# An attention and MoE kernel: heads laid out in four classes, the 64-row attention products in turns over four 64x64 quarters in place of two

## What is computed

```python
# attention, per head: state is 48 x 48
k_n = k / (norm(k) + 1e-6)
for t in range(768):
    y[t] = q[t] @ state
    v_old = k_n[t] @ state
    state = state + beta[t] * outer(k_n[t], v[t] - v_old)
# first MoE, all 3072 tokens, 384 -> 768 -> 384
x = maximum(maximum(y @ w1, y @ w2), y @ w3) @ w_out
# second MoE: noisy gate, top 2 of 8 experts, 384 -> 1024 -> 384
```

## Time and profile before

| | |
|---|---|
| median of 3 runs | 1016.75 us (1013.34 to 1016.77) |
| profiled execution, span from first to last instruction | 1010.6 us |
| TensorE busy | 990.2 us, 98% of the span |
| VectorE, ScalarE, GpSimd busy | 727.5, 464.6, 218.4 us |
| share of the chain that ended last | TensorE 92%, VectorE 3%, ScalarE 2% |
| mean granted TensorE clock | 0.989 |

### The profile page before, as it was taken

One profiled execution on the slowest core, in us unless ns is written; L12 is line 12 of the kernel. 1 busy time (PEld: TensorE's weight loads), 2 busy tenths in 40 slices (PEclk: granted clock), 3 DMA queues, 4 the chain that ended last, 5 costly groups with the idle time before them and its releaser, 6 DMA issues.

```text
span 1010.6 us, 26075 instructions
## 1 busy us (share of the span) xinstructions
PE 990.2 (98%) x10597; PEld 920.7 (91%) x10597; DVE 727.5 (72%) x1705; ACT 464.6 (46%) x696; POOL 218.4 (22%) x235
## 2 busy tenths in 40 slices
PE   8999999999999999999999999999999999999995
PEld 7688898898898898898999999999999999999995
DVE  7878797786895885435578777767777677776872
ACT  4543245234225324223455556545565465655551
POOL 0484400220210220222044122121121212212111
PEclk7899999999999999999999999999999999999998
DMA  9450321510420330235654535253352516525121
GB/s 315 124 113 2 96 54 34 146 37 24 133 60 3 95 77 3 73 124 181 246 206 115 163 51 162 43 144 77 47 168 56 163 38 172 177 61 155 36 30 23
DMA packets 71191, 101.70 MB, mean 101 GB/s; under 512 B 28608, under 2 KB 59584, under 8 KB 70720
## 3 DMA queue, kind: packets, MB, share of 16 engines
q1 hardware_dynamic: 59024, 78.10, 25.4%
q0 software_dynamic: 10992, 20.70, 10.6%
q10 hardware_dynamic: 1088, 1.65, 0.5%
HBM read 136.98 MB, written 29.51 MB: 165 GB/s over the span
## 4 chain that ended last, share of the span: by engine, by line
PE 92%; DVE 3%; ACT 2%; issue 1%; DMA 1%; POOLq 0%; SPq 0%; POOL 0%; DVEq 0%; ACTq 0%
PE ps L2051 44%; PE ps L2214 19%; PE ps L2099 8%; PE ps L1849 4%; PE ps L2225 3%; PE ps L1977 2%; PE ps L2009 2%; PE ps L1827 2%; PE ps L2115 2%; PE ps L1998 2%; PE ps L1907 1%; PE ps L1946 1%; DMA w1s<-in_we 1%; PE ps L1957 1%; PE ps L2201 1%
## 5 line engine op out<-in xcount | busy, mean ns | idle before, releaser
L2051 PE MATMUL ps<-xr,wr_in 128*128 128x512 f32 x972 | 234.1, 395 | 0.3 <-ACT xr L960 0.3
L2051 PEld LDWEIGHTS ps<-xr,wr_in 128*128 128x128 f32 x972 | 179.2, 188 | 39.3 <-issue 0.3
L2051 PE MATMUL ps<-xbT,w1r 128*128 128x256 f32 x1728 | 211.6, 283 | 0.5
L2051 PEld LDWEIGHTS ps<-xbT,w1r 128*128 128x128 f32 x1728 | 209.7, 192 | 2.4 <-issue 2.1
L2214 PE MATMUL ps<-w2r,hbT 128*128 128x384 f32 x1152 | 205.9, 336 | 0.0
L2214 PEld LDWEIGHTS ps<-w2r,hbT 128*128 128x128 f32 x1152 | 198.9, 188 | 0.0
L782 POOL DMA_INDIRECT out_rows<-yb,idx x55 | 89.8, 1633 | 376.4 <-DVE yb L1627 289.8
L1037 ACT ACTIVATE hbT<-ps 128x512 fp32r<-128x512 f32 x96 | 57.3, 597 | 168.5 <-PE ps L2051 168.5
L1439 DVE TENSOR_TENSOR w1r<-w1s,w1r 128x768 fp32r<-128x768 f32 x124 | 117.4, 956 | 17.8 <-ACT w1r L1021 15.7
L1021 ACT CAST w1r<-w1s 128x768 fp32r<-128x768 f32 x124 | 101.1, 827 | 25.4 <-DMA w1s<-in_we 25.4
L1609 DVE SCALAR_TENSOR_TENSOR hbT<-ps,hbT 128x512 fp32r<-128x512 f32 x96 | 66.1, 691 | 62.9 <-ACT hbT L1037 62.8
(11 more groups left out here) (253 smaller groups left out, 1127.6 us busy)
## 6 DMA issues: line engine op xcount, KB each, us to landing
w1s<-in_we SPq DMA_DIRECT2D x31, 1536.0 KB
w2s<-in_we SPq DMA_DIRECT2D x31, 1536.0 KB
xb<-rows SPq DMA_DIRECT2D x24, 402.0 KB, 3.6
kv_s<-in_kv SPq DMA_DIRECT2D x24, 384.0 KB, 3.6
k_s<-in_k SPq DMA_DIRECT2D x12, 512.0 KB, 4.3
joint<-in_q SPq DMA_DIRECT2D x24, 256.0 KB, 5.0
out_rows<-padrow SPq DMA_DIRECT2D x13, 384.0 KB, 4.6
w_in<-in_w_blocks SPq DMA_DIRECT2D x3, 1152.0 KB, 11.3
```

The lines of the kernel that those rows point to most:

```text
L2051: mm = pe.matmul(dst, w, m, start=(opens and n == 0), stop=(closes and n == len(todo) - 1))
```

## The change

- On the host, `columns` lays out keys and queries so that the dimensions of the heads of batches 0 and 1 lie in one row half and those of batches 2 and 3 in the other, whatever h is. With the tokens in half h, that gives four classes of heads. `dim_half(a)` is the half of pair a, `dim_slot(h, a)` its place in it.
- `quarters(one)` issues one product of each class in turn. The products of `gram` (all but chunk 1), `k_state_and_q`, `first_k_q`, `solve_u` (from chunk 2) and `state_step` (all but chunk 1) go through it, each class into a quarter of its own.
- State and u of a head lie in the same buffer only for two of the four classes (they are in different row halves there). For the other two, state and u are in the same row half of two buffers: their outputs are made by two products into one place, `state_output` and `token_output`, in turns over four quarters. The others stay whole (`whole_output`), in turns over two column halves. So `outputs` issues 48 products in place of 32. In chunks 0 and 1 the half `n = 0` changes in the same way over two quarters.
- ScalarE: `u_out` makes four copies of 64x384 in place of two of 64x768 (from chunk 2); `y_out` makes two copies as before, with other places.

```diff
+        def quarters(one):
+            for i in range(HP):
+                one(1, i)
+                one(0, HP + i)
+                one(0, i)
+                last = one(1, HP + i)
+            return last
+        def dim_slot(h, a):
+            return (1 - h) * HP + a % HP
+        def dim_half(a):
+            return 1 - a // HP
...
             def u_out(c):
...
-                for h_ in range(2 if c else 1):
-                    nc.scalar.copy(by_bank_pair(state_u(c, h_, tokens(h_))), token_products(h_)).then_inc(s_u, 1)
+                for h_ in range(2):
+                    for g in range(2):
+                        last = nc.scalar.copy(u_half_rows(c, h_, g), half_products(D_BANKS, (h_ + g) % 2, h_))
+                    last.then_inc(s_u, 1)
...
             # k_state_and_q
                 def one(h, a):
+                    rows, n = dims(dim_half(a)), dim_slot(h, a)
                     return pe.matmul(ps[tokens(h), C_BANKS + a // 4, a % 4 * (D + L):(a % 4 + 1) * (D + L)],
-                                     k_s[c % 4][dims(h), a], joint[c % 2][h][dims(h), a], start=True, stop=True)
-                turns(one).then_inc(p_rp, 1)
+                                     k_s[c % 4][rows, n], joint[c % 2][dim_half(a)][rows, n], start=True, stop=True)
+                quarters(one).then_inc(p_rp, 1)
...
             # solve_u
-                    return pe.matmul(ps[rows, D_BANKS + a // HP, a % HP * D:a % HP * D + D],
+                    place = (rows, D_BANKS + a // HP) if c < 2 else (tokens((h + a // HP) % 2), D_BANKS + h)
+                    return pe.matmul(ps[place[0], place[1], a % HP * D:a % HP * D + D],
...
             # state_step
-                    return pe.matmul(ps[dims(h), first + a // HP, a % HP * D:a % HP * D + D],
+                    return pe.matmul(ps[dims(dim_half(a)), first + 1 - h, a % HP * D:a % HP * D + D],
...
             def outputs(c):
-                outputs_of(c, 0, D_BANKS)
-                outputs_of(c, 1, D_BANKS).then_inc(p_y, 1)
+                for i in range(HP // 2):
+                    a = i // 2 * NP + i % 2
+                    heads = ((0, a), (1, HP + a + 2), (0, a + 2), (1, HP + a))
+                    for h, n in heads:
+                        state_output(c, y_place(h, n), h, n)
+                    for h, n in heads:
+                        token_output(c, y_place(h, n), h, n, False)
+                for i in range(HP // 2):
+                    a = i // 2 * NP + i % 2
+                    for h in range(2):
+                        whole_output(c, y_place(h, (1 - h) * HP + a), h, (1 - h) * HP + a)
+                        mm = whole_output(c, y_place(h, (1 - h) * HP + a + 2), h, (1 - h) * HP + a + 2)
+                mm.then_inc(p_y, 1)
...
     def columns(t):
-        wide = np.zeros((C, 2, L, B, NP, L), dtype=np.float32)
-        wide[:, ::-1, 0:D] = t.reshape(B, NP, 2, C, L, D).transpose(3, 2, 5, 0, 1, 4)
+        wide = np.zeros((C, 2, L, 2, B // 2, NP, L), dtype=np.float32)
+        wide[:, :, 0:D, ::-1] = t.reshape(2, B // 2, NP, 2, C, L, D).transpose(4, 0, 6, 3, 1, 2, 5)
```

More of the change, by code:

```diff
@@ L947, in y_out @@
                 act.wait_ge(p_xT, c // 2 * 2)
-                for h_ in range(2):
-                    nc.scalar.copy(y_rows(c, h_), token_products(h_)).then_inc(s_y, 1)
+                for half in range(2):
+                    nc.scalar.copy(y_columns(c, half), y_products(half)).then_inc(s_y, 1)
             def x_high(cp):
@@ L1868, in one @@
                 def one(h, a):
+                    rows, n = dims(dim_half(a)), dim_slot(h, a)
                     return pe.matmul(ps[tokens(h), H_BANKS + a // HP, a % HP * L:a % HP * L + L],
-                                     k_s[0][dims(h), a], joint[0][h][dims(h), a, D:], start=True, stop=True)
-                turns(one).then_inc(p_rp, 1)
+                                     k_s[0][rows, n], joint[0][dim_half(a)][rows, n, D:], start=True, stop=True)
+                quarters(one).then_inc(p_rp, 1)
             def blocks_to_rows():
@@ L1986, in solve_u @@
                 else:
-                    turns(one).then_inc(p_u, 1)
+                    quarters(one).then_inc(p_u, 1)
             def state_step(c, halves=(0, 1)):
@@ L2005, in outputs_of @@
-            def outputs_of(c, n, first):
-                def one(h, a):
-                    rows = slice(0, P if h else L + D)
-                    return pe.matmul(ps[tokens(h), first + a // HP, a % HP * D:a % HP * D + D],
-                                     joint[c % 2][h][rows, a, D:], joint[c % 2][h][rows, a, 0:D], start=True, stop=True)
-                return half_turns(one, n)
-            def outputs(c):
-                outputs_of(c, 0, D_BANKS)
-                outputs_of(c, 1, D_BANKS).then_inc(p_y, 1)
+                if halves == (0, 1):
+                    quarters(one).then_inc(p_s, 1)
+                else:
+                    for n in halves:
+                        mm = half_turns(one, n)
+                    if 1 in halves:
+                        mm.then_inc(p_s, 1)
@@ new lines, in whole_output, with state_output @@
+            def whole_output(c, place, h, a):
+                rows = slice(0, P if h else L + D)
+                return pe.matmul(place, joint[c % 2][h][rows, a, D:], joint[c % 2][h][rows, a, 0:D],
+                                 start=True, stop=True)
+            def state_output(c, place, h, a):
+                rows, n = dims(1 - h), dim_slot(h, a)
+                return pe.matmul(place, joint[c % 2][1 - h][rows, n, D:], joint[c % 2][1 - h][rows, n, 0:D],
+                                 start=True, stop=False)
@@ new lines, in token_output, with place @@
+            def token_output(c, place, h, a, opens):
+                rows = tokens(h)
+                return pe.matmul(place, joint[c % 2][h][rows, a, D:], joint[c % 2][h][rows, a, 0:D],
+                                 start=opens, stop=True)
+            def outputs_of(c, n, first):
+                def place(h, a):
+                    return ps[tokens(h), first + a // HP, a % HP * D:a % HP * D + D]
+                if n:
+                    return half_turns(lambda h, a: whole_output(c, place(h, a), h, a), n)
+                for i in range(HP):
+                    heads = ((1, HP + i), (0, i))
+                    if c:
+                        for h, a in heads:
+                            state_output(c, place(h, a), h, a)
+                    for h, a in heads:
+                        mm = token_output(c, place(h, a), h, a, c == 0)
+                return mm
```

25 lines of the change are left out of this document (17 added, 8 removed).

## The result

The changed kernel takes **997.5 us** (median of 4 runs, 994.2 to 999.01) against 1016.76 before: ratio **0.983, 95% interval [0.981, 0.985]**. The same file run again (experiment 7) gave 0.981 [0.979, 0.983]. The stated range of 976 to 1003 holds the time, but the forecast of 988 is 9.5 us too low, and the forecast's own range (981 to 995) does not hold it: 997.5 is nearer to rival 2's 1000. The profiled span fell from 1010.6 to 992.3.

The account below looks back on a forecast made before the run. TensorE's queue was taken to bound the kernel until another engine's chain. Savings 3.8+2.1+17.0+5.75 = 28.6 took the span from 1010.6 to 982.0, plus 6.15 gave 988 us; own range 981 to 995, 8-in-10 range 976 to 1003.

Parts of the forecast that it names:

- rival 2: Clock falls in the new waits before state steps, 1.7 us lost each, seven times: +12, 1000 us; chance 0.17.
- What bounds, and the pace of four quarters: TensorE's queue bounds steady passes; with four quarters k call 3.21 to 1.67 us, u 2.00 to 1.07, Grams 3.88 to 2.0.
- 1.04 us per 64 records [...] is a floor of the queue: From 32x32 products taking the same at both clocks: TensorE's queue goes no faster, so state step 1.57 to 1.04 us.
- Steady passes, forecast -17.0: Three attention passes, -5.65 us each of the 7.6 that TensorE's queue sheds; ScalarE's u copies make it wait.
- Last pass, forecast -5.75: Final attention pass, no Grams and no root: two each of k, u and state step savings, less 0.26 us for outputs.
- First pass, forecast -2.1: First attention pass: Grams' 1.88 us lost to VectorE, 2.5 us saved by TensorE turn into a wait.
- After it 0.53+1.54 are kept and the second half is held by VectorE's state step: First pass, after the first state step: state step and k product savings stay, giving -2.1 us.
- Start, forecast -3.8: Before the passes: first Gram -0.9, work up to VectorE's inverse -2.7 in all, second chunk's k product and outputs -1.1 us.
- rival 3: Weight loads on the same rows do not overlap: u, state step, Gram gain nothing; sum -3.5, 1013 us; chance 0.08.
- rival 4: Tiles on the same columns do not overlap: nothing saved, added products cost +10.5, 1027 us; chance 0.10.
- Rival 1: All savings kept, no wait on VectorE or ScalarE: 40 us less, 977 us; chance 0.12.

Follow-up runs that it names:

- experiment 7: Changed kernel with one h product put between dense calls: 1011.36 us, ratio 0.992; beside it the changed kernel unedited on another chip: 994.71 us, 0.981.
- experiment 4: Changed kernel with ScalarE's first u copies of each pass ahead of the root and the square-root table loaded before them: 1002.35 us, ratio 0.984.
- experiment 5: Kernel of experiment 4 with VectorE's second state of the first pass also moved ahead of its steps of the inverse: 994.59 us, ratio 0.981.
- the 64 products (alone): Changed kernel with 64 products of 64x64 on a constant in TensorE's wait between the second and third Gram: 995.22 us, ratio 0.979.
- the run with 32 products: Changed kernel with 32 products of 64x64 on a constant in TensorE's wait between the second and third Gram: 1003.48 us, ratio 0.986.
- experiment 1: Changed kernel with the four-quarter calls in the old order, 16 products over each pair of quarters, layout kept: 1009.96 us, ratio 0.9957 to the kernel before.
- experiments 3 to 5: The first: changed kernel with u copies ahead of ScalarE's root or cast, 1000.66 us, ratio 0.985; the others are experiment 4 and experiment 5.

## Why the prediction was right, and where it was off

That the time lies in the stated range is in part luck: two shortfalls that the forecast has not (the packet waits, and the first pass held by VectorE) are covered by a range made for waits and falls of the clock.

**What bounds, and the pace of four quarters: right.** Calls as forecast within 0.03 us, but for the state step: the step that failed is "1.04 us per 64 records [...] is a floor of the queue". It ran 64 records in 0.75 to 0.90. So there is no such floor; the row it was read from has a scattered stationary, which is the likely cause of its 57 ns for four and is not shown at full clock. So a call takes 0.1 to 0.3 us less than forecast, and the two steady passes without a packet wait came out 0.1 and 0.4 us below their forecast.

**Steady passes, forecast -17.0, measured -13.7.** Two of them gave -6.07 and -5.76 (forecast -5.65) and the middle one -1.84. The waits on ScalarE were as worked out. The 3.9 us that it lacks against them are, within 0.1, the two packet waits (0.77 and 1.36) and what a stretch at half clock right behind the second costs:

```profile
253.49:256.90 3.41, 3.41 (x10) 2.63 (x9) 1.49 (x9) 1.37 (x3) 0.07 (x1) 0.50 0.53 120
```

3.41 us at half rate are 1.7 lost. The set run again has the same waits and the same loss (77.01 us).

**Last pass, forecast -5.75, measured -4.8**: 0.59 is a packet wait in its outputs, the other 0.4 stays open.

**First pass, forecast -2.1, measured +0.4.** The failed step is "After it 0.53+1.54 are kept and the second half is held by VectorE's state step". All of it is held, the first half's gain too: experiment 4 took the wait of 2.36 us away and the pass was no shorter; experiment 5 moved VectorE's state and it was 2.7 shorter, 71.46 us where the kernel before took 73.78. Two stretches of 3.4 us at half clock (93.06 and 113.54, behind waits of 1.15 and 2.36) and a packet wait of 1.19 lie in it too; with the end set by VectorE they need not cost anything, which no run shows apart.

**Start, forecast -3.8, measured +0.3** in the profile, within a spread of 5 us over profiles. The calls did become shorter (L1909 1.99 us in place of 3.68), but the clock was at half rate for 17.1 us as before and for 10.2 more (41.86 to 52.10), behind two waits of 0.4 us that were not there before (one for VectorE, one for a packet); at that clock the second chunk's k product took 2.8 us and not 1.7. Two more packet waits that the kernel before has not lie in it: 1.02 us in u at 42.18 and 1.02 in the state step at 62.22. How much of it is clock, how much packets and how much chance is open.

**Rival 2 came true in part.** It was priced at 12 us with seven falls; the profile has four beyond those of before, 20.5 us at half clock. The timed runs agree: the mean granted clock was 0.986 for the kernel before and 0.975 to 0.977 for the changed one, and among runs of the kernel before 0.01 of clock goes with 3.2 to 6.4 us. By that estimate, from runs that differ in clock by chance and not on purpose, the clock is 3 to 7 of the 9.5 us that the forecast was low. With the 64 products (alone) the clock was 0.986 again, and the ratio 0.979. In the passes it fell behind waits of 1.15, 2.36 and 1.36 us, but not behind one of 1.19 at 131.10, nor in either profile of the changed kernel behind the 0.93 us before each first state step, which are the waits that the rival meant. In the run with 32 products it fell behind none of the first pass's waits (1.13, 2.37 and 1.71 us). And the row on which the rival was priced, 1.44 us at 30.71, was a packet wait itself. The Trainium skill, "TensorE: Matmul & The Clock Gate", Part 1, What's actually happening, ties the gate to how busy the engine has been lately, which fits the falls; which wait brings one and which does not, the rows here do not tell.

**Rivals 3 and 4: refuted**, rival 4 by the k calls (1.69 us, not over 3) and by experiment 1 (same columns), rival 3 by u and the Grams, which took half their time, and by the state step, whose neighbours in the order share their rows half of the time and which ran fastest. The Trainium skill, "TensorE: Matmul & The Clock Gate", Part 3, The mechanism, lets weight loads overlap running matmuls only where the row group differs; the 0.75 us for 64 records do not bear it out.

**Rival 1** fell with the waits on ScalarE, as forecast; experiments 3 to 5 show that they can't simply be moved.

## What to carry to other kernels

When a change lets an engine run the same instructions in half the time, ask next what feeds it instructions: 128 matmul records (64 small products) in 2 us outran the reading of the program, at places that depend on how the code falls into packets. Cost a stage by the engine that releases its end; a faster TensorE in a pass whose end waits for VectorE's queue is worth nothing, and the place of one instruction in that queue was worth more than the whole change there. And a wait of 1 to 2 us that a change opens can have a second price, 1.7 us here for each 3.41 us at half clock where TensorE binds; not every such wait brought a fall.

## What the hardware showed that was not expected

- A packet of TensorE's program holds 127 or 128 matmul records; where calls are dense, TensorE waits for it 0.3 to 3.2 us (up to 1.4 in the attention passes of the changed kernel) and goes on 1.2 to 1.6 us behind its landing.
- Two products in a row for each quarter cost 0.15 us in 1.76: the others go on meanwhile.
- One chip of at least three shows holes of 0.35 to 0.63 us at fixed products of dense calls, at a granted clock of 1.00. Their cause is open.
- One code's start varied between 63.9 and 69.1 us.
